# One list of single-expert blocks instead of two, added to zeroed output rows, with gated weights in the gathered payload

## The reference

```python
# 1. causal convolution over 7 taps with softmax weights per head -> x
# 2. soft mixture: 8 experts with 4 slots each (32 slots)
logits = x @ phi
d = softmax(logits, axis=0); c = softmax(logits, axis=1)
slot_out = relu((d.T @ x) @ w1[e]) @ w2[e]     # per expert e, its 4 slots
x = c @ slot_out
# 3. top-2 mixture: 8 experts, hidden size 1024
noisy = x @ w_gate + log1p(exp(x @ w_noise)) * noise
top2, top2_w = two largest, softmax of the two
out[t] = sum over k of top2_w[t, k] * relu(x[t] @ w1[e_k]) @ w2[e_k]
```

## Time and profile before

| | |
|---|---|
| runs, median of 3 | 973.6 us (973.33 to 973.91) |
| the profiled execution, own time | 979.98 us |
| its span in the profile | 978.1 us |
| granted TensorE clock, mean over the span | 0.945 |
| TensorE busy | 905.8 us (93%) |
| VectorE busy | 625.6 us (64%) |
| ScalarE busy | 452.3 us (46%) |
| GpSimd busy | 341.7 us (35%) |
| first gather of the expert stage | 358.8 us into the span |

### The profile page before, as it was taken

The page is one execution under the profiler, slowest core; times in us unless marked ns, Lnnn a source line. Parts: engine busy times, 40 slices in busy tenths (PEclk is TensorE's granted clock), DMA queues, the critical chain, the costliest instruction groups (busy, mean ns, idle before and its releaser), DMA issues.

```text
span 978.1 us, 26085 instructions
## 1 busy us (share of the span) xinstructions
PE 905.8 (93%) x7930; PEld 726.2 (74%) x7931; DVE 625.6 (64%) x1398; ACT 452.3 (46%) x971; POOL 341.7 (35%) x362
## 2 busy tenths in 40 slices
PE   5999989996787679999999999999999999999995
PEld 5999979993463337878777777777777777777774
DVE  5132343346478968888776777677767777777773
ACT  2222221231041445555565666566656655665563
POOL 5000000001001022433455555555555656565652
PEclk9999989998656689999999999999999999999998
DMA  7447777887645212333333333333334444444441
GB/s 238 130 130 219 205 247 199 258 282 203 192 112 135 97 44 81 95 94 98 107 109 111 108 111 106 111 109 110 107 109 109 115 106 110 104 111 113 109 116 30
DMA packets 76908, 129.07 MB, mean 132 GB/s; under 512 B 10764, under 2 KB 45532, under 8 KB 74936
## 3 DMA queue, kind: packets, MB, share of 16 engines
q1 hardware_dynamic: 60696, 110.35, 38.3%
q0 software_dynamic: 15248, 17.49, 8.8%
q10 hardware_dynamic: 912, 0.52, 0.2%
HBM read 63.49 MB, written 16.86 MB: 82 GB/s over the span
## 4 chain that ended last, share of the span: by engine, by line
PE 87%; DVE 4%; DMA 4%; issue 2%; ACT 1%; POOL 0%; another core or an unknown queue 0%; ACTq 0%; SPq 0%; PEldq 0%; DVEq 0%
PE ps L1494 31%; PE ps L1498 15%; PE ps L1473 11%; PE ps L1229 10%; PE ps L1278 4%; PE ps L1280 4%; PE ps L1448 3%; PE ps L1222 3%; PE ps L1463 2%; DMA a_room<-in_moe_w 1%; PE ps L1375 1%; DMA lg<-in_moe_w 1%; PE ps L1394 1%; PE ps L1322 1%; DMA gate_room<-in_moe_w 1%
## 5 line engine op out<-in xcount | busy, mean ns | idle before, releaser
L681 ACT ACTIVATE x_ring<-ps 128x512 f16<-128x512 f32 x472 | 256.3, 598 | 215.3 <-PE ps L1473 188.2
L1494 PE MATMUL ps<-w2hl,x_ring 128*128 x1888 | 347.3, 327 | 1.1 <-DVE x_ring L1172 0.8
L1162 DVE SCALAR_TENSOR_TENSOR x_ring<-ps,x_ring 128x512 f16<-128x512 f32 x472 | 303.1, 684 | 11.5 <-ACT x_ring L681 5.1
L1494 PEld LDWEIGHTS ps<-w2hl,x_ring 128*128 128x128 f16 x1888 | 176.4, 97 | 97.8 <-issue 7.4
L553 POOL DMA_INDIRECT stage<-pay_rows,row_id x151 | 150.3, 995 | 275.9 <-PE ps L1473 159.2
L1498 PE MATMUL ps<-w2hl,x_ring 128*128 x1888 | 194.6, 246 | 1.1 <-DVE x_ring L1162 1.1
L563 POOL DMA_INDIRECT out_rows<-x_ring,row_id x151 | 169.8, 1125 | 58.4 <-issue 43.9
L1498 PEld LDWEIGHTS ps<-w2hl,x_ring 128*128 128x128 f16 x1888 | 163.1, 98 | 31.9 <-DVE x_ring L1162 1.9
L1473 PE MATMUL ps<-c,x_ring 96*128 96x128 f16 x1888 | 145.6, 220 | 0.5 <-DVE c L1155 0.5
L1155 DVE COPY c<-ps 96x256 f16<-96x256 f16 (+1 forms) x151 | 39.0, 258 | 143.7 <-PE ps L1463 124.8
L1473 PEld LDWEIGHTS ps<-c,x_ring 96*128 96x128 f16 x1888 | 122.6, 98 | 0.9 <-issue 0.9
(11 more groups left out here) (310 smaller groups left out, 658.6 us busy)
## 6 DMA issues: line engine op xcount, KB each, us to landing
x_ring<-a_room SPq DMA_DIRECT2D x236, 192.0 KB
x_ring<-in_x SPq DMA_DIRECT2D x14, 1536.0 KB, 6.9
stage<-in_moe_w SPq DMA_DIRECT2D x24, 768.0 KB, 9.6
a_room<-in_moe_w SPq DMA_DIRECT2D x12, 768.0 KB, 11.5
gate_room<-in_moe_w SPq DMA_DIRECT2D x8, 768.0 KB, 10.1
stage<-pay_rows,row_id POOLq DMA_INDIRECT x151
out_rows<-x_ring,row_id POOLq DMA_INDIRECT x151
pay_rows<-x_ring SPq DMA_DIRECT2D x1, 1904.0 KB, 6.0
```

What stands on the lines that cost most here:

```text
L681: a.activation(hh[:, m % 2, 4 * half:4 * half + 4, :].rearrange("p j q -> p (j q)"), ps[:, 2 + 2 * (m % 2) + half, :], ACT.Relu).then_inc( ...
L1162: last = v.scalar_tensor_tensor(hl[:, m % 2, 4 * half:4 * half + 4, :].rearrange("p j q -> p (j q)"), ps[:, 2 + 2 * (m % 2) + half, :], 0. ...
L1494: t_.matmul(ps[:, 6 + b % 2, 0:2 * D], hh[:, m % 2, j, :], w, start=k == 0 and j == 0, stop=False)
```

## The change

1. One list. `LB` becomes 61: a list of 61 single-expert blocks in which a left-over token stands twice, once for each of its experts. `PRE = 24`, `NBK = 146`, `NPASS = 231`. The list's places are summed over both of a class's experts (more entries in `cls_m`), the 14 lookups have 122 columns in place of 66, and one `list_table` comes at the end. It also makes `list_src`, twice the row number plus one where the place is that of the other expert.
2. Payload rows of 64 values, both halves already multiplied by their gates: GpSimd does two products of 128 x 3584 values (the 32 weights of each token by its gate). SyncE writes each half on its own, in stretches of 32 values (128 B). ScalarE's copy into `cg` goes. A pair block gathers whole rows of 256 B, a single block half rows of 128 B. The splits no longer multiply, and are one instruction for both experts.
3. Zeroed output. ScalarE issues five transfers that write zeros over all of `out_rows` (14848 rows of 768 B), between `a_low` and the exponential `m_exp`.
4. All single blocks add to the output; each waits for the scatter of the single block before it. The first scatter waits for the zeroing.
5. One room for a late w1 load is `a3_room` in place of `lg`, and that load waits for `so_ps` in place of `cg_ready`.

```diff
-    LB = (N - FP * P + (E - 1) * (P - 1)) // P
-    PRE = FP - 2 * LB
-    NBK = FP + 2 * LB
-    NPASS = 2 * NBK - 2 * LB
+    LB = (2 * (N - FP * P) + E * (P - 1)) // P
+    PRE = FP - LB
+    NBK = FP + LB
+    NPASS = 2 * FP + LB
-    KP = NS + 2
+    KP = 2 * NS
...
+        c_all_rows = lg[:, PAD:PAD + T, :]
+        c_gated = [ring[:, 0:T * NS].rearrange("p (t s) -> p t s", s=NS), c_all_rows]
... SyncE
-            sp.wait_ge(gates_ready, 2)
-            sp.dma_start(pay[0:N, :].rearrange("(p t) k -> p t k", t=T), cg[:, :, :]).then_inc(pay_out, 16)
+            for k in range(2):
+                sp.wait_ge(gates_ready, k + 1)
+                sp.dma_start(pay[0:N, k * NS:(k + 1) * NS].rearrange("(p t) s -> p t s", t=T), c_gated[k]
+                             ).then_inc(pay_out, 16)
... GpSimd
+            pool.wait_ge(c_ready, 1)
             step(g.tensor_scalar(gm[:, 0, :], gm[:, 3, :], C_SCALE, None, ALU.mult))
             step(g.tensor_tensor(gm[:, 1, :], gm[:, 0, :], gm[:, 2, :], ALU.mult))
             for k in range(2):
                 step(g.tensor_tensor(pr[:, 3, :], pr[:, 5 + k, :], gm[:, 0, :], ALU.mult))
                 step(g.tensor_tensor(pr[:, 4, :], pr[:, 6 - k, :], gm[:, 1, :], ALU.mult))
-                g.tensor_tensor(cg[:, :, NS + k], pr[:, 3, :], pr[:, 4, :], ALU.add).then_inc(gates_ready, 1)
+                step(g.tensor_tensor(gm[:, 4 + k, :], pr[:, 3, :], pr[:, 4, :], ALU.add))
+                g.tensor_tensor(c_gated[k], c_all_rows, gm[:, 4 + k, :].unsqueeze(2).to_broadcast([P, T, NS]), ALU.mult
+                                ).then_inc(gates_ready, 1)
                 pool.wait_ge(gates_ready, k + 1)
...
             def scatter(n):
-                if n == PRE + 2 * LB + 1:
-                    for s in range(4):
-                        pool.wait_ge(y_out[s], 16 * ((n - 1 - s) // 4 + 1))
+                if n == 0:
+                    pool.wait_ge(out_zero, 16 * 5)
+                if not is_pair(n) and n > PRE + 1:
+                    pool.wait_ge(y_out[(n - 2) % 4], 16 * ((n - 2) // 4 + 1))
                 pool.wait_ge(y_ready, n + 1)
-                second_list = dict(compute_op=ALU.add) if not is_pair(n) and list_no(n) == 1 else {}
+                added = {} if is_pair(n) else dict(compute_op=ALU.add)
... ScalarE
-            a.activation(cg[:, :, 0:NS], lg[:, PAD:PAD + T, :], ACT.Copy).then_inc(cg_ready, 1)
...
             a_low(E // 2 - 1)
+
+            act.wait_ge(consts, 1)
+            part = T // 4
+            for k in range(4):
+                act.dma_start(out[0:N, :].rearrange("(p t) d -> p t d", t=T)[:, k * part:(k + 1) * part, :],
+                              zero16[:, 0:2 * D].bitcast(F32).unsqueeze(1).to_broadcast([P, part, D])
+                              ).then_inc(out_zero, 16)
+            act.dma_start(out[N:ROWS, :].rearrange("(p a) d -> p a d", a=4),
+                          zero16[:, 0:2 * D].bitcast(F32).unsqueeze(1).to_broadcast([P, 4, D])).then_inc(out_zero, 16)
             act.wait_ge(m_diff, 1)
             a.activation(gm[:, 2, :], gm[:, 2, :], ACT.Exp).then_inc(m_exp, 1)
...
-                for k in (range(2) if is_pair(b) else range(1)):
-                    gate = NS + (k if is_pair(b) else 1 - list_no(b))
-                    last = a.activation(csp[:, b % 4, k, 0:2, :],
-                                        crow[:, b % CR, 0:NS].unsqueeze(1).to_broadcast([P, 2, NS]), ACT.Copy,
-                                        scale=crow[:, b % CR, gate:gate + 1])
-                last.then_inc(cs_hi, 1)
+                n = 2 if is_pair(b) else 1
+                a.activation(csp[:, b % 4, 0:n, 0:2, :], gated_rows(b).unsqueeze(2).to_broadcast([P, n, 2, NS]), ACT.Copy
+                             ).then_inc(cs_hi, 1)
... VectorE
-                for k in (range(2) if is_pair(b) else range(1)):
-                    gate = NS + (k if is_pair(b) else 1 - list_no(b))
-                    last = v.scalar_tensor_tensor(csp[:, b % 4, k, 2, :], crow[:, b % CR, 0:NS],
-                                                  crow[:, b % CR, gate:gate + 1], csp[:, b % 4, k, 0, :],
-                                                  ALU.mult, ALU.subtract)
-                last.then_inc(cs_lo, 1)
+                n = 2 if is_pair(b) else 1
+                v.tensor_tensor(csp[:, b % 4, 0:n, 2, :], gated_rows(b), csp[:, b % 4, 0:n, 0, :], ALU.subtract
+                                ).then_inc(cs_lo, 1)
```

More of the change, by code:

```diff
@@ L214, in soft_then_top2_moe @@
         in_class = place(LN, NCL)
-        list_past = place(2 * LB, NCL).rearrange("p (x b) -> p x b", x=2)
+        list_past = place(LB, NCL)
         lpos_f = place(2 * LN)
@@ L219, in soft_then_top2_moe @@
         tab_h = place(LN).bitcast(F16).rearrange("p (a n) -> p a n", a=2)
-        ltab = place(2 * LB).rearrange("p (a b) -> p a b", a=2)
-        lid = place(LB)
+        ltab, ltab_lo = (gates[:, 2 * F + i * 2 * LB:2 * F + (i + 1) * 2 * LB].rearrange("p (a b) -> p a b", a=2)
+                         for i in range(2))
+        lid, is_hi = (gates[:, 2 * F + (4 + i) * LB:2 * F + (5 + i) * LB] for i in range(2))
         hot1L = gates[:, 0:LB * HG].bitcast(F16).rearrange("p (s h b t) -> p s h b t", s=2, h=2, t=HH)
@@ L342, in all_blocks, with gated_rows @@
                 blk(0, b)
-            with eng.Fori(0, HPASS) as i:
+            with eng.Fori(0, LPASS) as i:
                 for b in range(PRE, PRE + 8):
                     blk(i, b)
-            for b in range(PRE + 8 * HPASS, LOFF):
+            for b in range(PRE + 8 * LPASS, NBK):
                 blk(0, b)
[L348 to L352, removed]
+        def gated_rows(b):
+            return crow[:, b % CR, 0:KP if is_pair(b) else NS].rearrange("p (k s) -> p k s", s=NS)
         def turns(i, b, slots):
@@ L459, in _ @@
             sp.wait_ge(list_eid, 1)
-            with sp.Fori(0, (NPASS - first_list) // 4) as i:
-                for m in range(first_list, first_list + 4):
+            with sp.Fori(0, (NPASS - known) // 4) as i:
+                for m in range(known, known + 4):
                     copy_a(i, m)
+            for m in range(known + (NPASS - known) // 4 * 4, NPASS):
+                copy_a(0, m)
         @block.gpsimd
@@ L572, in _ @@
                 ahead = n + CR - 2
[L573 to L574 removed]
+                if ahead == PRE + 1:
+                    pool.wait_ge(list_ready, 2)
                 if ahead < NBK:
@@ L847, in _ @@
             hi_c, lo_c = cls_col[:, 0:1], cls_col[:, 1:2]
-            first_hi, first_lo, step_lo, first_lo_up = (cls_col[:, j:j + 1] for j in range(2, 6))
+            first_hi, first_lo, step_lo = (cls_col[:, j:j + 1] for j in range(2, 5))
             step(v.scalar_tensor_tensor(lo_c, hi_c, -1.0, hi_c, ALU.add, ALU.mult))
@@ L876, in _ @@
             dve.wait_ge(hilo_ps, 1)
-            for x in range(2):
-                other, mine = ps[0:NCL, 3, x * NCL:(x + 1) * NCL], cls_col[:, x:x + 1]
-                step(v.tensor_scalar(cls_m[:, 3 * x, :], other, mine, None, ALU.is_equal))
-                step(v.tensor_tensor(cls_m[:, 3 * x + 1, :], cls_m[:, 3 * x, :], tri[0:NCL, 0:NCL], ALU.mult))
-                step(v.tensor_scalar(cls_m[:, 3 * x + 2, :], other, mine, cls_col[:, 2 + x:3 + x], ALU.is_gt, ALU.mult))
+            hi_of, lo_of = (ps[0:NCL, 3, x * NCL:(x + 1) * NCL] for x in range(2))
+            step(v.tensor_scalar(lo_row[:, :], lo_of[0:1, :], 1.0, None, ALU.min))
+            step(v.tensor_scalar(cls_m[:, 1, :], hi_of, hi_c, None, ALU.is_equal))
+            step(v.scalar_tensor_tensor(cls_m[:, 0, :], hi_of, lo_c, cls_m[:, 1, :], ALU.is_equal, ALU.add))
+            step(v.tensor_tensor(cls_m[:, 1, :], cls_m[:, 1, :], tri[0:NCL, 0:NCL], ALU.mult))
+            step(v.tensor_scalar(cls_m[:, 2, :], hi_of, hi_c, first_hi, ALU.is_gt, ALU.mult))
+            step(v.tensor_scalar(cls_m[:, 4, :], lo_of, lo_c, None, ALU.is_equal))
+            step(v.scalar_tensor_tensor(cls_m[:, 3, :], lo_of, hi_c, cls_m[:, 4, :], ALU.is_equal, ALU.add))
+            step(v.tensor_tensor(cls_m[:, 4, :], cls_m[:, 4, :], tri[0:NCL, 0:NCL], ALU.mult))
+            step(v.scalar_tensor_tensor(cls_m[:, 4, :], lo_of, hi_c, cls_m[:, 4, :], ALU.is_equal, ALU.add))
+            step(v.tensor_scalar(cls_m[:, 5, :], lo_of, hi_c, first_hi, ALU.is_gt, ALU.mult))
             dve.wait_ge(so_ps, E)
```

94 lines of the change are left out of this document (43 added, 51 removed).

## The result

The changed kernel takes 1013.72 us (median of 4 runs, 1012.82 to 1015.98) against 973.52 us: a ratio of 1.041, 95% interval 1.0393 to 1.0427, 40 us more. The profiled execution has a span of 1011.6 us, 33.5 us more than the one of before. Single executions of one kernel differ by some us here, so the 40 is told from the medians and the stages from the traces.

What follows compares the result with a forecast made beforehand. It took TensorE passes to bound the expert stage, and before it one chain from ScalarE's exponential to the first gather. The sum -12.6 + 40.7 + 14.0 = +42.1 on 973.6 gave 1016 us, 8-in-10 range 965 to 1050.

Steps and rivals of the forecast that it cites:

- cheap-rows rival: Zero rows from SBUF cost only their bytes: 23 us hold, payload hidden, table binds; +22, 996 us; chance 0.14.
- Part 3, the hold on ScalarE: Five zeroing issues ahead of the exponential hold ScalarE and delay the chain behind it by 40.7 us (2.3 to 48).
- 805 rows: Zero rows per DMA engine, of 928, that must go before ScalarE is free; priced at 50.6 ns each.
- Part 4, the lock: GpSimd's products of about 8 us block VectorE through a shared port; table of rows 11.5 us later (3 to 22).
- Part 4, the writes: Payload halves in 128 B stretches take 24.0 us each, landing after the table; first gather 14.0 us later, port stall included.
- Part 1, the passes: Expert stage: 236 passes become 231 at 2.51 us each, saving 12.6 us; wider lookups cost 0.
- its upper bound of 2.6 us: Most that widening the lookups from 66 to 122 columns could cost: 56 columns / 2.4 GHz x 112.
- Part 2, adding scatters: Expert stage: all single blocks adding, with their waits, cost 0, hidden by GpSimd's idle time; 61 us if uncovered.
- the held issues: Sign of being right: five issues on ScalarE's queue, four of which hold for about 8 to 11 us each.
- the late exponential: Sign of being right: ScalarE's exponential runs about 41 us later.
- the cast as long as a product: Sign of being right: a VectorE cast lasts as long as one GpSimd product of about 8 us.
- the payload landing after the table: Sign of being right: both payload writes land later than the table, at about 372 against 369 us without the hold.

Runs made afterwards that it cites:

- e1: The changed kernel with the zeroing of the output left out: 977.7 us, ratio 0.9995 to the kernel before.
- e4: The kernel before with only the five zeroing transfers added, at the same place on ScalarE: 1015.28 us, ratio 1.0384.
- e6: The changed kernel with zeroing spread early, no GpSimd products, and payload halves of 33 values (32 ungated weights and a gate): 1014.57 us, ratio 1.049.
- e11: The changed kernel with zeroing spread early, 128 B payload stretches 132 B apart, and an early transfer zeroing the payload: 1017.22 us, the kernel before 974.38.
- e5: The changed kernel with zeroing spread early and GpSimd's two products left out (ungated payload halves): 962.95 us, ratio 0.9947 to the kernel before.
- e10: The changed kernel with early zeroing, contiguous 35-value payload (ungated weights, both gates, their difference), VectorE selecting single blocks' gates: 965.55 us, ratio 0.9907 to the kernel before.

## Why the prediction was right

Forecast 1016 us, measured 1013.7. No rival's time was met, though the cheap-rows rival had one thing right that the forecast had not: the payload is hidden and the table binds. The sum met the result better than its terms did.

- **Part 3, the hold on ScalarE:** predicted 40.7 us, measured 38.4, and e1 and e4 show that it is the whole loss. ScalarE was held as SyncE had been in the earlier trace rows. But the 40.7 is right by two errors. The zeros moved at 310 GB/s, faster than the 243 of the loads from DRAM: 39.6 ns a row and not 50.6, so 805 rows are 32 us, 8.9 less. The rest can be read from the window of the hold. From 305.15 to 344.10 the DMA engines moved 303 GB/s, 11.8 MB; 1.7 MB of that were the twelve a3 copies and the payload's zero rows, which SyncE issued in the same stretch and which my sum had left out: 5.5 us at 310 GB/s. The other 10.1 MB are 822 rows an engine, so the 805 was nearly right (0.7 us).
- **Part 4, the lock:** predicted 11.5 us for products of 8 us, measured 7.7 for products of 6.23. The same two VectorE operations were held as foretold, the cast and L1011's comparison. The Trainium skill ("SBUF — State Buffer", "Who interferes with whom") names casts and tensor_scalar operations among those that can take the pair of ports shared with GpSimd, and clears an instruction with at most one SBUF input outside the two-port modes. The trace agrees: the operations from PSUM between the two ran in their old time. Over-sized was the price per value: with the measured 6.23 us for 3584 values and the 0.42 us for 112, a value costs 1.67 ns and not 2, with 0.23 us fixed (no row had given the 0.2 that I took).
- **Part 4, the writes: the step that failed.** "From the row price above: 22 ns + 128 B" gave 24.0 us a half and made the payload late. A stretch of 128 B cost 11.8 ns, so a half took 10.6 us of transfer, both landed 22 us before the table and not 3 us behind it, and the table set the first gather. Instead of 14.0 us the first gather lost 7.7. The price was carried from reads of DRAM rows to writes of DRAM, which no row of the kernel before had shown in small stretches. The price of the Trainium skill ("DMA: Bandwidth & Descriptors", "Why small descriptors are slow"), about 3 cycles a packet and by my estimate 7.5 us a half, was nearer here; e6 and e11 show writes of about that size far above it.
- **Part 1, the passes:** 5 x 2.51 = 12.6 us went, the repeats took 7.51 us. "so the width is below what bounds one: I take 0" failed, and so did its upper bound of 2.6 us: 14 lookup steps cost 0.4 us each more (0.92 against 0.52 us), 5.6 us. I priced a column at one cycle, from dense operands. So a gain of 7.0 us was due. Seen were 8.1 in the mean of three pairs, or 7.8 without the first two passes; the last us is not explained.
- **Part 2, adding scatters:** 0, as predicted; an adding issue takes 1.57 us of GpSimd, and in the single-block part TensorE kept 49.6 to 50.0 of every 50 us.

The errors: hold -2.3, first gather -6.3, expert stage +4.5 (8.1 instead of 12.6), together -4.1 us; 42.1 - 4.1 = 38.0, and the interval of the ratio is 38.3 to 41.6 us. The two large ones had opposite signs, and within the hold a row price 8.9 us too high stood against 5.5 us of copies that were left out. The near hit is luck to that extent. What did carry it is that ScalarE's hold was read from SyncE's rows. Of the signs named beforehand, the held issues, the late exponential and the cast as long as a product came; the payload landing after the table did not.

Open: why e5, the same path up to the first gather as e10, came out at 0.9947 and not 0.991 (the intervals, 0.9928 to 0.9966 and 0.989 to 0.9923, do not meet). It still wrote two halves and gathered rows of 256 B; no run separated these, and they ran on different chips. And a single execution of one kernel scatters by some us, so no pair of traces fixes the expert stage to better than that.

## What to carry to other kernels

Look at what stands behind an issue of transfers on its engine. Here one transfer alone was taken in 0.43 us, even one of 2688 KB; each one behind it held the engine for 6 to 14 us, until most of what was in front had moved. Spread fills over a stage in which each issue finds the one before it landed, and look at the landing times: the 3.7 MB that e11 added in an early stage landed late and kept loads waiting. Price an operation on GpSimd also by what VectorE has to do beside it, and a lookup by the stride of what it streams.

## What was not expected of the hardware

- **Stretches of 128 B written to DRAM:** 11.8 ns each per engine where they start at multiples of 128 B (174 GB/s over the core); with the same length but starts 132 B apart the two writes landed in 37.3 and 66.4 us instead of 12.5 and 15.4 (46 GB/s in a window of the writes alone), and stretches of 132 B moved at 43 GB/s. No run tried other distances.
- **A moving operand with its fp16 values four apart:** 122 columns cost 117 ns in the chain, dense 55 ns; the changed kernel's own eight lookups of 122 give 115 ns (0.92 / 8), and 66 strided columns 65 ns (0.52 / 8). From 66 to 122 columns that is (115 - 65) / 56 = 0.89 ns a column, 2.1 cycles at the granted 2.4 GHz.
